# Two fused MLPs behind a dynamic convolution: steps 0 and 1 of the first MLP woven, closing products split around lone up parts

## The chip, the cores and the metric

The kernel runs on one core of a Trainium2 chip. The metric is the device time of one execution in microseconds, median of the runs.

## What is computed

A per-token convolution (softmax over 7 taps per head, 8 heads of 24 features), then two MLPs of 192 to 2048 to 192 features, the first with a leaky ReLU, the second with an ELU, over 8192 tokens:

```
w = softmax(weight_gen, axis=-1)                  # [2, 4096, 8, 7]
out[b,s,h,:] = sum_k w[b,s,h,k] * x_pad[b,s+k,h,:]  # x_pad: 6 zero rows ahead
x = out.reshape(8192, 192)
h = x @ moe_w_in;   g = maximum(0.01*h, h);            x = g @ moe_w_out
h = x @ moe2_w_in;  g = where(h > 0, h, exp(min(h, 0)) - 1);  out = g @ moe2_w_out
```

## The kernel before

Each f32 factor of a matrix product is held as two rounded parts, high and low (`*_hi`, `*_lo`), so that a product becomes three. The 192 features are held as 128 (`_a`) and 64 (`_b`); of the 64, the high part lies in partitions 0 to 63 and the low part in 64 to 127 of one tile `in_b`, and `in_b_up` holds the high part once more in the upper half. Most products use one half of TensorE's rows (LOW, HIGH), and two such, one in each half, run side by side: "a pair" here.

**Chunks, phases, steps.** Tokens come in 16 chunks of 512. A phase is one MLP on one chunk; the order is MLP 1 of chunk 0 (phase 0), MLP 1 of chunk 1 (phase 1), MLP 2 of chunk 0 (phase 2), and then in turn. A phase has 8 steps of 256 hidden features; step number g = 8 x phase + s. One step is an *up* part (up products into the PSUM bank pair `hidden[:, s % 2]`), an activation on ScalarE (line 1091 or 1093), a rounding to `hid_hi` on ScalarE (line 1109), the rest `hid_lo` on VectorE (line 1380), and three steps later a *down* part that adds into `y_a` and `y_b`.

**TensorE's order** is written out in `phase` (line 896). The up part has a first half (5 pairs) and a second half (4 pairs). The second half waits on `s_open` for the last product of the first, since both add to the same banks. In an ordinary step `down_open` (4 pairs) stands between the two halves, the second half is interleaved with down products, and `down_close` (line 766, 4 pairs) ends the step. In three steps the up part is *lone*, its halves back to back: steps 2, 8 and 10. Step 0 is `up_first` (line 669) and step 1 `up_whole` (line 695), in whole-array products. Ahead of step 8 stand the down part of step 5, the transposes of chunk 1's mix (line 877), and the whole down part of step 6 (`down_alone`, line 778).

**Waits that matter.** The up part of step g overwrites the bank pair of step g - 2: it waits for that step's activation (`s_leak`) where g - 2 is in `ASIDE` = (0, 1, 2, 9), and for its `hid_lo` (`s_lo` at least g - 1) otherwise. Step 0's `in_b` products wait at line 686 for `s_xin` 2 (VectorE, line 1299), step 8 at line 913 for `s_xin` 4 (VectorE, line 1302). In phase 0 a step with even s waits for the splits of its quarter of the up weights (`s_uplo`).

**Other engines.** ScalarE (line 1186 on): issues the load of `wk[1]`, two exponentials, packs, rounds the weight quarters 0 and 1 of `w_in` (`round_up`, lines 974 and 980), makes the input's high parts, rounds down weights (`round_down`, line 990), then runs the steps; `first_step` (line 1111) activates step 0 in two halves, rounds it and then rounds quarter 2. VectorE makes the mix of chunk 0 (`first_mixing`, line 1228; the newest tap is `product(6, prod, 0, J)`, line 1240), the low parts of inputs and weights, and every `hid_lo`. GpSimd makes the other mixes. SyncE's queue (line 443 on) loads `wk[0]`, the rows of `x`, waits for all of them (lines 449 and 450), loads quarters 0 and 1 of `w_in` and the first of `w_out`, and behind `s_termv` and `s_unpack` (lines 455 and 457) the rest.

Of the kernel before, what the change touches and what calls it, by code (L numbers as in the profile page):

```python
# [5 lines left out]
def attention_leaky_elu_mlps(  # L6
# [61 lines left out]
    with ctx:  # L68
# [345 lines left out]
        def _(sp):  # L414
# [28 lines left out]
            load_w(0)  # L443
            sp.dma_start(xw[:, PAD:, :], x_rows[:, 0:J * D].rearrange("p (j d) -> p j d", d=D)).then_inc(s_x0, 16)
# [155 lines left out]
        def _(pe):  # L600
# [68 lines left out]
            def up_first():  # L669

                def product(i, w, v, **flags):
                    return nc.tensor.matmul(hidden[:, 0, HALF[i]], w[0][:, i * P:(i + 1) * P], v[input_of(0, 0)][:, :], **flags)


                pe.wait_ge(s_xhi, 1)
                pe.wait_ge(s_uplo, 1)
                for i in (0, 1):
                    product(i, up_a_hi, in_a_hi, start=True, stop=False)
                    product(i, up_a_lo, in_a_hi, start=False, stop=False)

                pe.wait_ge(s_xin, 1)
                product(0, up_a_hi, in_a_lo, start=False, stop=False)
                product(1, up_a_hi, in_a_lo, start=False, stop=False)
# [3 lines left out]
                product(0, up_b_hi, in_b, start=False, stop=False)  # L687
                product(1, up_b_hi, in_b, start=False, stop=False)
                pe.wait_ge(s_uplo, 2)
                pe.wait_ge(s_xup, 1)  # L690
                low, high = up_pair(0, input_of(0, 0), 0, stop=True)
                low.then_inc(s_up1, 1)
                high.then_inc(s_up, 1)

            def up_whole(m, src, s):

                def product(i, w, v, **flags):
                    cols = slice((2 * s + i) * P, (2 * s + i + 1) * P)
                    return nc.tensor.matmul(hidden[:, s % 2, HALF[i]], w[m][:, cols], v[src][:, :], **flags)  # L699

                up_pair(m, src, s, start=True)
                for i in (0, 1):
                    product(i, up_a_hi, in_a_hi, start=False, stop=False)
                    product(i, up_a_lo, in_a_hi, start=False, stop=False)
                    product(i, up_a_hi, in_a_lo, start=False, stop=False)
                    product(i, up_b_hi, in_b, start=False, stop=True).then_inc(s_up if i else s_open, 1)
# [59 lines left out]
            def down_close(m, s, d):  # L766

                down_a(m, s, d, LOW, 0, 2)
                pe.wait_ge(s_ybfirst, d + 1)
                down_b(m, s, d, HIGH, 0, 0)  # L770
                down_a(m, s, d, LOW, 1, 0)
                down_b(m, s, d, HIGH, 0, 1)
# [716 lines left out]
```

## Time and profile before

| | |
|---|---|
| median of 3 runs | 1130.13 us (1129.84 to 1130.41) |
| the profiled execution | 1129.72 us |
| its span, first to last instruction | 1127.9 us |
| TensorE busy | 1119.7 us, 99% of the span |
| ScalarE, VectorE, GpSimd busy | 744.0, 624.5, 390.4 us |
| mean granted TensorE clock | 0.999 |

In the profile PE is TensorE (PEld its weight loads), ACT ScalarE, DVE VectorE, POOL GpSimd, SP SyncE. L609 is line 609 of the kernel. A matmul record lasts longer (0.39 us) than the distance to the next one, since they are pipelined: waits of TensorE are read from the distance between starts. What stands behind "<-" in brackets is the inferred releaser of an idle time, and can be another that ended at the same moment.

### The profile page before, as it was taken

The numbers are of one execution on the slowest core, as the hardware profiler recorded it, in microseconds if no ns is written. First come the engines' busy times: TensorE is split into PE (matmuls) and PEld (weight loads), VectorE is DVE, ScalarE is ACT, GpSimd is POOL, SyncE is SP. The second block draws the span as 40 slices with busy tenths as digits, with TensorE's granted clock in tenths as the row PEclk, the third lists the DMA queues.
The fourth block names the chain that finished last, engine by engine and source line by source line (L and its number), as shares of the span: only waits on it lengthen the run. The fifth ranks groups of instructions, "written<-read, shape, count | busy, mean of one in ns | idle before, by whom it ended". The sixth has DMA issues, their size and how long they took to land.

```text
span 1127.9 us, 22691 instructions
## 1 busy us (share of the span) xinstructions
PE 1119.7 (99%) x9794; PEld 921.8 (82%) x9794; DVE 624.5 (55%) x654; ACT 744.0 (66%) x837; POOL 390.4 (35%) x407
## 2 busy tenths in 40 slices
PE   8999999999999999999999999999999999999998
PEld 6888888888888888888888888888888888888886
DVE  8677547365463645636456364554736546363555
ACT  6577657576575766757567575765757657576676
POOL 6663622607135080440805317062260713500000
PEclk9999999999999999999999999999999999999999
DMA  5412020211202102021020201102021120110001
GB/s 173 119 50 85 17 81 15 82 29 29 82 1 82 29 28 83 1 82 29 29 82 3 88 22 57 54 19 83 11 82 29 29 82 2 43 29 29 15 1 57
DMA packets 46080, 54.88 MB, mean 49 GB/s; under 512 B 4254, under 2 KB 34718, under 8 KB 45980
## 3 DMA queue, kind: packets, MB, share of 16 engines
q1 hardware_dynamic: 45836, 53.30, 15.6%
q8 instruction: 78, 1.28, 0.5%
q14 instruction: 22, 0.18, 0.1%
q10 hardware_dynamic: 144, 0.11, 0.0%
HBM read 35.71 MB, written 17.69 MB: 47 GB/s over the span
## 4 chain that ended last, share of the span: by engine, by line
PE 98%; DVE 1%; ACT 0%; DMA 0%; issue 0%; DVEq 0%
PE y_a L730 31%; PE hidden L609 31%; PE y_b L713 21%; PE hidden L614 10%; PE hidden L665 5%; DMA wk<-in_weight_gen_dram 0%; PE hidden L699 0%; DVE prod L1233 0%; DVE act L1233 0%; PE y_b L856 0%; DVE mix L1233 0%; PE hidden L666 0%; DVE staged L1233 0%; DVE act L1236 0%; DVE raw_d L1233 0%
## 5 line engine op out<-in xcount | busy, mean ns | idle before, releaser
L730 PE MATMUL y_a<-hid_hi,dn 64*128 64x512 f32 x2048 | 625.5, 386 | 0.0
L730 PEld LDWEIGHTS y_a<-hid_hi,dn 64*128 64x128 f32 x2048 | 375.7, 184 | 40.0
L713 PE MATMUL y_b<-hid_hi,dn 64*128 64x512 f32 x1024 | 395.5, 386 | 0.0
L713 PE MATMUL y_b<-hid_lo,dn 64*128 64x512 f32 x1024 | 395.4, 386 | 0.0
L730 PE MATMUL y_a<-hid_lo,dn 64*128 64x512 f32 x1024 | 394.4, 386 | 0.0
L609 PE MATMUL hidden<-in_a_hi,up_a_hi 64*128 64x512 f32 x1016 | 294.1, 387 | 0.2
L609 PE MATMUL hidden<-in_a_lo,up_a_hi 64*128 64x512 f32 x1016 | 293.6, 386 | 0.0
L609 PE MATMUL hidden<-in_a_hi,up_a_lo 64*128 64x512 f32 x1016 | 293.6, 386 | 0.0
L614 PE MATMUL hidden<-in_b,up_b_hi 64*128 64x512 f32 x1016 | 293.6, 386 | 0.0
L1380 DVE TENSOR_TENSOR hid_lo<-hidden,hid_hi 128x1024 fp32r<-128x1024 f32 x124 | 151.6, 1222 | 255.0 <-ACT hid_hi L1109 255.0
L1380 DVE TENSOR_TENSOR hid_lo<-act,hid_hi 128x1024 fp32r<-128x1024 f32 x131 | 165.5, 1264 | 189.2 <-ACT hid_hi L1109 189.2
L1091 ACT ACTIVATE hidden<-hidden 128x1024 f32<-128x1024 f32 x124 | 125.0, 1008 | 196.0 <-PE hidden L614 196.0
L1093 ACT ACTIVATE act<-hidden 128x1024 f32<-128x1024 f32 x127 | 130.5, 1027 | 159.8 <-PE hidden L614 158.1
L384 POOL TENSOR_TENSOR mix<-xw,wk 128x384 f32<-128x384 f32 x30 | 26.5, 884 | 562.6 <-DVE wk L1287 562.5
L713 PEld LDWEIGHTS y_b<-hid_hi,dn 64*128 64x128 f32 x1024 | 188.4, 184 | 20.3 <-issue 0.2
L730 PEld LDWEIGHTS y_a<-hid_lo,dn 64*128 64x128 f32 x1024 | 188.5, 184 | 20.0
L713 PEld LDWEIGHTS y_b<-hid_lo,dn 64*128 64x128 f32 x1024 | 188.5, 184 | 19.9
L397 POOL TENSOR_TENSOR mix<-mix,prod 128x384 f32<-128x384 f32 x180 | 194.3, 1079 | 2.4
L1355 DVE SCALAR_TENSOR_TENSOR act<-act,hidden 128x1024 f32<-128x1024 f32 x129 | 155.6, 1206 | 45.7 <-ACT act L1098 45.3
L384 POOL TENSOR_TENSOR prod<-xw,wk 128x384 f32<-128x384 f32 (+1 forms) x182 | 171.9, 952 | 9.4
L609 PEld LDWEIGHTS hidden<-in_a_hi,up_a_hi 64*128 64x128 f32 x1016 | 140.4, 184 | 22.0 <-PE hidden L666 1.5
L614 PEld LDWEIGHTS hidden<-in_b,up_b_hi 64*128 64x128 f32 x1016 | 140.4, 184 | 19.9
(143 smaller groups left out, 1312.3 us busy)
## 6 DMA issues: line engine op xcount, KB each, us to landing
xw<-in_x_dram SPq DMA_DIRECT2D x14, 960.0 KB, 5.2
raw_b<-squares_out SPq DMA_DIRECT2D x60, 96.0 KB, 2.2
out_dram<-staged SPq DMA_DIRECT2D x15, 384.0 KB, 2.6
squares_in<-prod SPq DMA_DIRECT2D x56, 96.0 KB, 2.0
squares_out<-ya SPq DMA_DIRECT2D x15, 256.0 KB, 2.0
raw_a<-squares_in SPq DMA_DIRECT2D x14, 256.0 KB, 2.9
raw_d<-in_moe_w_out_dram SPq DMA_DIRECT2D x8, 384.0 KB, 3.4
squares_out<-yb SPq DMA_DIRECT2D x15, 128.0 KB, 2.2
```

What stands on the lines that cost most here:

```text
L384: product = ops.tensor_tensor(dst, src, w, ALU.mult)
L397: ops.tensor_tensor(mix[:, j0:j1, :], mix[:, j0:j1, :], terms[k % n][:, j0:j1, :], ALU.add).then_inc(done, 1)
L609: return nc.tensor.matmul(hidden[:, s % 2, HALF[i]], w[m][rows, cols], v[src][rows, :], start=start, stop=stop)
L614: return nc.tensor.matmul(hidden[:, s % 2, HALF[i]], up_b_hi[m][rows, cols], in_b[src][rows, :], start=False, stop=stop)
L665: low = nc.tensor.matmul(hidden[:, s % 2, HALF[0]], up_b_lo[m][LOW, cols], in_b[src][LOW, :], start=start, stop=stop)
L713: return nc.tensor.matmul(y_b[d // ST % 2][:, :], dn[m][rows, f, P:2 * P], v[rows, s % HB, HALF[i]], start=start, stop=stop)
L730: return nc.tensor.matmul(y_a[bank][:, :], dn[m][rows, f, w:w + P], v[rows, s % HB, HALF[i]], start=start, stop=stop)
L1091: nc.scalar.activation((act if g in ASIDE else hidden)[:, s % 2, :], hidden[:, s % 2, :], ACT.Prelu, alpha=SLOPE).then_inc(s_leak, 1)
L1093: nc.scalar.activation(act[:, s % 2, :], hidden[:, s % 2, :], ACT.Relu, scale=-1.0).then_inc(s_relu, 1)
L1355: nc.vector.scalar_tensor_tensor(out=a, in0=a, scalar=-1.0, in1=h, op0=ALU.add, op1=ALU.max).then_inc(done, 1)
L1380: nc.vector.tensor_tensor(hid_lo[:, s % HB, :], (act if m or g in ASIDE else hidden)[:, s % 2, :], hid_hi[:, s % HB, :].bitcast(f32), ALU. ...
```

## The change

- SyncE's queue issues the load of `wk[1]` directly behind that of `wk[0]`; ScalarE's queue no longer does.
- `up_first` and `up_whole` become `up_first_two`: the high-input products of step 1 stand ahead of the wait for `in_b`, the others behind step 0's last. Step 1's `b_lo` pair (`up_pair`) goes between the halves of step 2's up part and signals `s_up` for step 1.
- `down_close` can be issued in halves. Step 6's stands between the halves of step 8's up part; of step 7's the first half (2 pairs) stays in step 9 and the second (2 pairs) stands between the halves of step 10's.
- ScalarE rounds quarter 2 of the up weights ahead of step 0's activation instead of behind its rounding.

```diff
--- before.py
+++ after.py
@@ -441,6 +441,7 @@
 
 
             load_w(0)
+            load_w(1)
             sp.dma_start(xw[:, PAD:, :], x_rows[:, 0:J * D].rearrange("p (j d) -> p j d", d=D)).then_inc(s_x0, 16)
             sp.wait_ge(s_pad, 1)
             for to in HALO_ROWS:
@@ -666,44 +667,41 @@
                 high = nc.tensor.matmul(hidden[:, s % 2, HALF[1]], up_b_lo[m][HIGH, cols], in_b_up[src][HIGH, :], start=start, stop=stop)
                 return low, high
 
-            def up_first():
-
-                def product(i, w, v, **flags):
-                    return nc.tensor.matmul(hidden[:, 0, HALF[i]], w[0][:, i * P:(i + 1) * P], v[input_of(0, 0)][:, :], **flags)
-
+            def up_first_two():
+                src = input_of(0, 0)
+
+                def product(s, i, w, v, **flags):
+                    cols = slice((2 * s + i) * P, (2 * s + i + 1) * P)
+                    return nc.tensor.matmul(hidden[:, s, HALF[i]], w[0][:, cols], v[src][:, :], **flags)
+
+                def a_hi(s):
+                    for i in (0, 1):
+                        product(s, i, up_a_hi, in_a_hi, start=True, stop=False)
+                        product(s, i, up_a_lo, in_a_hi, start=False, stop=False)
+
+                def a_lo(s):
+                    for i in (0, 1):
+                        product(s, i, up_a_hi, in_a_lo, start=False, stop=False)
 
                 pe.wait_ge(s_xhi, 1)
                 pe.wait_ge(s_uplo, 1)
-                for i in (0, 1):
-                    product(i, up_a_hi, in_a_hi, start=True, stop=False)
-                    product(i, up_a_lo, in_a_hi, start=False, stop=False)
-
+                a_hi(0)
                 pe.wait_ge(s_xin, 1)
-                product(0, up_a_hi, in_a_lo, start=False, stop=False)
-                product(1, up_a_hi, in_a_lo, start=False, stop=False)
+                a_lo(0)
+                a_hi(1)
 
                 pe.wait_ge(s_uphi, 2)
                 pe.wait_ge(s_xin, 2)
-                product(0, up_b_hi, in_b, start=False, stop=False)
-                product(1, up_b_hi, in_b, start=False, stop=False)
+                for i in (0, 1):
+                    product(0, i, up_b_hi, in_b, start=False, stop=False)
                 pe.wait_ge(s_uplo, 2)
                 pe.wait_ge(s_xup, 1)
-                low, high = up_pair(0, input_of(0, 0), 0, stop=True)
+                low, high = up_pair(0, src, 0, stop=True)
                 low.then_inc(s_up1, 1)
                 high.then_inc(s_up, 1)
-
-            def up_whole(m, src, s):
-
-                def product(i, w, v, **flags):
-                    cols = slice((2 * s + i) * P, (2 * s + i + 1) * P)
-                    return nc.tensor.matmul(hidden[:, s % 2, HALF[i]], w[m][:, cols], v[src][:, :], **flags)
-
-                up_pair(m, src, s, start=True)
-                for i in (0, 1):
-                    product(i, up_a_hi, in_a_hi, start=False, stop=False)
-                    product(i, up_a_lo, in_a_hi, start=False, stop=False)
-                    product(i, up_a_hi, in_a_lo, start=False, stop=False)
-                    product(i, up_b_hi, in_b, start=False, stop=True).then_inc(s_up if i else s_open, 1)
+                a_lo(1)
+                product(1, 0, up_b_hi, in_b, start=False, stop=False)
+                product(1, 1, up_b_hi, in_b, start=False, stop=False).then_inc(s_open, 1)
 
             def down_b(m, s, d, rows, i, n):
 
@@ -763,13 +761,16 @@
                 down_a(m, s, d, LOW, 0, 1)
                 down_a(m, s, d, HIGH, 1, 2)
 
-            def down_close(m, s, d):
-
-                down_a(m, s, d, LOW, 0, 2)
-                pe.wait_ge(s_ybfirst, d + 1)
-                down_b(m, s, d, HIGH, 0, 0)
-                down_a(m, s, d, LOW, 1, 0)
-                down_b(m, s, d, HIGH, 0, 1)
+            def down_close(m, s, d, halves=(0, 1)):
+
+                if 0 in halves:
+                    down_a(m, s, d, LOW, 0, 2)
+                    pe.wait_ge(s_ybfirst, d + 1)
+                    down_b(m, s, d, HIGH, 0, 0)
+                    down_a(m, s, d, LOW, 1, 0)
+                    down_b(m, s, d, HIGH, 0, 1)
+                if 1 not in halves:
+                    return
                 down_a(m, s, d, LOW, 1, 1)
                 down_b(m, s, d, HIGH, 1, 0)
                 down_a(m, s, d, LOW, 1, 2)
@@ -896,8 +897,9 @@
             def phase(m, c, ph, dm, dc):
                 for s in range(ST):
                     g = ST * ph + s
-                    if known(ph) and g == 0:
-                        up_first()
+                    if g == 0:
+                        up_first_two()
+                    if g < 2:
                         continue
                     of, step = (dm, ST - LAG + s) if s < LAG else (m, s - LAG)
                     if ph == 1 and s == 0:
@@ -907,7 +909,9 @@
                         transpose_mix(1, 1)
 
                         pe.wait_ge(*down_split(0, DN_PARTS - 1))
-                        down_alone(0, ST - 2, g - 2)
+                        pe.wait_ge(s_lo, g - 1)
+                        down_open(0, ST - 2, g - 2)
+                        down_middle_apart(0, ST - 2, g - 2)
                     if s == 0:
 
                         pe.wait_ge(s_min if m else s_xin, 2 * (c + 1))
@@ -931,10 +935,14 @@
                     elif of_two == 1:
 
                         pe.wait_ge(s_g, ST * c_two + (s - 2) % ST + 1)
-                    if ph == 0 and s == 1:
-                        up_whole(m, input_of(m, c), s)
-                        continue
                     up(m, input_of(m, c), g, s, False)
+                    if g == 2:
+
+                        up_pair(0, input_of(0, 0), 1, stop=True)[1].then_inc(s_up, 1)
+                    if (ph, s) == (1, 0):
+                        down_close(0, ST - 2, g - 2)
+                    if (ph, s) == (1, 2):
+                        down_close(0, ST - 1, g - 3, (1,))
                     if (ph, s) in ((0, 2), (1, 0), (1, 2)):
                         up(m, input_of(m, c), g, s, True)
                         continue
@@ -955,7 +963,7 @@
                     else:
                         up(m, input_of(m, c), g, s, True)
                         down_middle_apart(of, step, d)
-                    down_close(of, step, d)
+                    down_close(of, step, d, (0,) if (ph, s) == (1, 1) else (0, 1))
 
             sum_first_mix()
             run(pe, phase)
@@ -1114,7 +1122,6 @@
                     nc.scalar.activation(act[:, 0, HALF[i]], hidden[:, 0, HALF[i]], ACT.Prelu, alpha=SLOPE).then_inc(signal(s_leak, s_leak1, i), 1)
                 act_e.wait_ge(s_leak1, 1)
                 rounding(0, 0, 0, 0)
-                round_up(0, 2)
 
             def last_step():
                 s = ST - 1
@@ -1183,7 +1190,6 @@
                         if (ph, s) in DN2_AT:
                             round_down(1, DN2_AT.index((ph, s)))
 
-            act_e.dma_start(wk[1][:, :, :], w_rows[:, J * H * TAPS:2 * J * H * TAPS].rearrange("p (a k) -> p a k", k=TAPS)).then_inc(s_w[1], 16)
             softmax_exp(0)
             softmax_exp(1)
 
@@ -1196,6 +1202,7 @@
             mlp1_input_hi(0, 1)
             round_up_b(0, 1)
             round_down(0, 0)
+            round_up(0, 2)
             run(act_e, phase)
             take_y(1, CH - 1, LAST)
             stage_last()
```

## Rows read from the trace of the kernel before

**Rows 1.** Stretches: us, busy PE, PEld, DVE, ACT, POOL, clock, DMA, GB/s.

```profile
61.70:1115.00 1053.30, 1053.30 (x9296) 870.70 (x9294) 570.67 (x587) 699.27 (x773) 353.67 (x364) 1.00 0.14 43
```

**Rows 2.** Timeline, TensorE, steps 0 to 3: start, us, line, output<-inputs, count.

```profile
16.84 0.73 PE L672 MATMUL hidden<-in_a_lo,up_a_hi 128*128 128x512 f32 x2
17.82 0.71 PE L672 MATMUL hidden<-in_b,up_b_hi 128*128 128x512 f32 x2 [0.25 <-ACT up_b_hi L980]
...
21.19 0.51 PE L609 MATMUL hidden<-in_a_hi,up_a_hi 64*128 64x512 f32 x2
...
22.70 0.50 PE L609 MATMUL hidden<-in_a_hi,up_a_hi 64*128 64x512 f32 x2
23.04 0.39 PE L609 MATMUL hidden<-in_a_hi,up_a_lo 64*128 64x512 f32 x2
...
23.74 0.39 PE L609 MATMUL hidden<-in_a_hi,up_a_hi 64*128 64x512 f32 x2
```

**Rows 3.** Timeline, VectorE, 4 to 40 us.

```profile
4.49 0.42 DVE L1264 TENSOR_REDUCE wsum<-soft 128x32 f32<-128x256 f32 x1 [0.16 <-ACT soft L1000]
...
14.13 0.68 DVE L1213 TENSOR_TENSOR up_a_lo<-raw_a,up_a_hi 128x512 fp32r<-128x512 f32 x1
...
16.82 0.86 DVE L1299 TENSOR_TENSOR in_b<-y_a,in_b 64x256 fp32r<-64x256 f32 x2
...
22.48 1.88 DVE L1380 TENSOR_TENSOR hid_lo<-act,hid_hi 128x1024 fp32r<-128x1024 f32 x1
...
30.36 1.22 DVE L1380 TENSOR_TENSOR hid_lo<-hidden,hid_hi 128x1024 fp32r<-128x1024 f32 x1 [0.47 <-ACT hid_hi L1109]
...
33.26 1.35 DVE L1213 TENSOR_TENSOR up_a_lo<-raw_a,up_a_hi 128x512 fp32r<-128x512 f32 x1
...
35.54 1.21 DVE L1380 TENSOR_TENSOR hid_lo<-hidden,hid_hi 128x1024 fp32r<-128x1024 f32 x1
```

**Rows 4.** Timeline, TensorE, into step 6.

```profile
36.48 0.39 PE L730 MATMUL y_a<-hid_lo,dn 64*128 64x512 f32 x1
...
36.90 0.50 PE L609 MATMUL hidden<-in_a_hi,up_a_hi 64*128 64x512 f32 x2
```

**Rows 5.** Timeline, TensorE, step 8, its two halves.

```profile
52.33 0.39 PE L665 MATMUL hidden<-in_b,up_b_lo 64*128 64x512 f32 x1
...
52.78 0.50 PE L609 MATMUL hidden<-in_a_hi,up_a_hi 64*128 64x512 f32 x2
```

**Rows 6.** Timeline, ScalarE, 14 to 34 us.

```profile
17.61 0.83 ACT L990 ACTIVATE dn<-raw_d 128x768 fp32r<-128x768 f32 x1
18.99 1.09 ACT L1114 ACTIVATE act<-hidden 128x512 f32<-128x512 f32 x2 [0.56 <-PE hidden L665]
...
21.14 0.61 ACT L974 ACTIVATE up_a_hi<-raw_third 128x512 fp32r<-128x512 f32 x1
...
24.46 1.03 ACT L1091 ACTIVATE act<-hidden 128x1024 f32<-128x1024 f32 x1 [0.18 <-DVE hid_lo L1380]
```

**Rows 7.** Timeline, SyncE's queue, 5 to 17 us.

```profile
6.86 0.34 SPq L421 DMA_DIRECT2D raw_a<-in_moe_w_in_dram  x1
...
13.70 1.26 SPq L427 DMA_DIRECT2D ya<-in_moe_w_in_dram  x2
```

**Rows 8.** The chain that ended last, its beginning: start, us, what.

```profile
0.72 2.48 DMA wk<-in_weight_gen_dram
...
5.82 1.99 DVE prod L1233 x3
```

**Rows 9.** Issue to landing: into ya at 12 to 17, wk after 60.

```profile
DMA to landing us min/median/max: 4.6/4.7/4.7
...
DMA to landing us min/median/max: 2.1/2.6/3.1
```

**Rows 10.** Timeline, VectorE, 46 to 60 us.

```profile
50.05 0.68 DVE L1302 TENSOR_TENSOR in_b<-hidden,in_b 64x512 fp32r<-64x512 f32 x1
56.12 1.22 DVE L1380 TENSOR_TENSOR hid_lo<-hidden,hid_hi 128x1024 fp32r<-128x1024 f32 x1 [5.39 <-ACT hid_hi L1109]
```

## The prediction

> **What bounds the kernel now.** I read the stretches first. From 61.7 to 1115 us TensorE is busy in every microsecond, at a granted clock of 1.00 [rows 1]. The change edits nothing in that stretch and nothing in the tail, and the stretch has no idle time to give. Both differences can only come from the first 61.7 us, and reach the end only as a shift of the whole stretch. So I asked, gap by gap, what ends each TensorE gap before 61.7 us, and whether that thing moves.
>
> Then the timeline of TensorE alone. In a run without a wait a pair of half-array products starts every 0.2275 us and a whole-array one every 0.235 us. After a wait the first one holds the second back to 0.34 us (22.70 to 23.04), 0.11 us more than the step: I call this the refill. Five gaps matter:
> - 17.82: the second of the two low-half products that start at 16.84 is due at 17.08, so the next was due at 17.31. Wait 0.51, refill about 0.09 [rows 2]. The profile hints at ScalarE's `up_b_hi`, but line 686 waits for `s_xin` 2, which VectorE's `in_b` subtraction gives at 16.82 + 0.86 = 17.68 [rows 3].
> - 22.70: step 2's second half waits for its own first half (`s_open`). The first half starts at 21.19, its fifth pair at 22.24; 22.70 is 0.46 later, so 0.23 of wait and 0.11 of refill [rows 2].
> - 36.90: step 6. The pair before started at 36.48, 0.42 earlier, so 0.19 of wait, and a refill of about 0.07 [rows 4]. This one is of another kind: step 6 needs `s_lo` 5, the rest of step 4, which VectorE starts at 35.54 and ends at 36.75 [rows 3].
> - 52.78: step 8's second half after its fifth pair at 52.33: 0.45, so 0.22 + 0.11 = 0.33 [rows 5].
> - the same again in step 10, two steps on, at the same size (0.33).
>
> **What sets 36.90** decides the first half of the change. Backwards on VectorE: 35.54 stands directly behind weight splits (33.26 and others) that follow 30.36, and 30.36 waits for ScalarE's `hid_hi` of step 3. ScalarE comes to that without a pause from 24.46 (activation of step 2, three roundings of weights, step 3), and 24.46 waits for VectorE's first `hid_lo` at 22.48 + 1.88 = 24.36, which stands in an unbroken VectorE queue back to the first product of the mix [rows 3, 6]. No link of this chain is a TensorE product of steps 0 to 2. So what TensorE gains before 24 us it waits for at 36.90.
>
> **The change part by part.**
>
> *wk[1]'s load moves from ScalarE's queue to SyncE's, second in order.* The x load and the halo loads are issued one issue later, about 0.4 us (SyncE's issues in [rows 7] take 0.34 and 0.63). SyncE issues the first MLP weights at 6.86, once the halo has landed; the VectorE product that needs it is the third of the group that starts at 5.82 and ends at 7.81, a quarter of a product long and so at about 7.4 [rows 7, 8]. With 0.4 the halo is there by 7.26: hidden, just. wk[1] would land about 1.13 + 2.6 = 3.7, and at the longest landing seen (3.1) at 4.2; VectorE takes it up just before 4.0 and has 0.16 us idle before 4.49 [rows 3], so it costs 0 to 0.16. wk[0] shares the engines with it less. Its landing took 2.48 and starts the critical chain; later loads of the same size took 2.1 to 3.1 [rows 8, 9]. So this part is worth between -0.38 and +0.16 on everything. I take -0.05, near nothing, because most of the 2.48 is common to all landings. The DMA page of the Trainium skill (DMA: Bandwidth & Descriptors, "Issuing engines are not separate DMA queues") says that transfers from either queue run on the same 16 engines interleaved, and that a second issuer saves only sequencer time. By that the part would be worth nothing but the 0.4 us of issue; no row here shows the two orders side by side.
>
> *Step 1 woven into step 0.* Four high-half products of step 1 (4 x 0.235 = 0.94) go into the 0.51 us wait before 17.82. The two `in_b` products of step 0 then start at 17.31 + 0.94 = 18.25, 0.43 later, and lose their refill, so step 0's result comes about 0.35 later and ScalarE's activation could start at 18.99 + 0.35 = 19.34 [rows 2, 6]. On TensorE alone the work behind is 0.60 us earlier. The switches between whole and half array are three before and three after, so they cancel.
>
> *round_up(0, 2) ahead of step 0 on ScalarE.* After `dn` at 17.61 (0.73 to the next) the two roundings start at 18.34 and 18.87, if the loads are there. The last of the third quarter's loads is issued at about 14.33 (the second of 13.70's pair) and lands 4.6 later, 18.95 [rows 7, 9]. So the second starts at 18.95 and ScalarE is free at 18.95 + 0.53 = 19.48 (call it S), or 19.9 if the landing slips with the 0.4 us of SyncE. The two halves of step 0's activation take 1.09, and TensorE sees them at S + 1.14.
>
> *Step 2 and the end of step 1.* Step 2's first half, due by TensorE at about 20.3, waits for that: S + 1.14 = 20.6 (before 21.19). Its fifth pair starts 1.05 later, step 1's last pair at +1.28 (it fills the `s_open` wait: gain 0.34), so `s_up` 2 gives ScalarE step 1 at S + 1.14 + 1.28 + 0.42 = S + 2.84. That takes 1.03, and step 3 needs it (`s_leak` 2): TensorE goes on at S + 3.89 = 23.4, before 23.74 [rows 2]. A gain of 0.34 is left of 0.94 (0.60 + 0.34), the rest turned into two new waits for ScalarE. ScalarE itself then rounds step 1 from S + 3.87 for 0.97, and is ready for step 2's activation at S + 4.84 = 24.32, against 24.46 where VectorE releases it [rows 6]. So the chain to 36.90 stays put with 0.14 us to spare; with S = 19.9 it slips by 0.28. I take +0.05, bounds 0 and +0.33. The 0.34 us that TensorE gained are waited for at 36.90.
>
> *Step 8: down_close of step 6 between the halves.* The four closing pairs fill 0.33 us. But they used to stand ahead of step 8's first half, and covered the wait for `s_xin` 4. That first half started at 52.33 - 4 x 0.2275 = 51.42; without four pairs ahead it is due at 50.51, while VectorE's `in_b` ends at 50.05 + 0.68 = 50.73 and reaches TensorE 0.05 to 0.14 later [rows 5, 10]. Both hang on the transposes of the second mix, so the distance is fixed whatever happens before. New wait about 0.30, new refill 0.11: 0.41 spent for 0.33 gained, net about +0.07. Bounds: -0.33 (no wait) and +0.2.
>
> *Step 10: half of down_close of step 7.* Two pairs fill the gap, 0.46 for 0.45, so the 0.33 is gained. The first half comes two pairs earlier, from about 58.15 (52.78 + 23 pairs and a refill) to 57.7; it needs the rest of step 8, 56.12 + 1.22 = 57.34 [rows 10], 0.3 us to spare. Net -0.33, at the worst -0.2. `s_dn` 7 and 8 come up to 2 us later; their readers (ScalarE's copy of `y_a` after step 9 and TensorE's step 11) come later still.
>
> Sum: -0.05 + 0.05 + 0.07 - 0.33 = **-0.26 us**. The profiled execution took 1129.72 (span 1127.9 and 1.8 around it); it would take 1129.46. The median of the runs lies 0.41 above that execution: **1129.9 us**. All lower ends together give -1.04, all upper ends +0.49.
>
> **The rivals.**
> - *The weave pays in full.* Every filled gap stays filled: -(0.60 + 0.34 + 0.33 + 0.33) = -1.6, 1128.5 us. For it: TensorE is the busy engine. Against it: 35.54 and 50.05, two VectorE rows that no edit moves [rows 3, 10]. Chance 0.07.
> - *No new wait in step 8*, otherwise as forecast: -0.26 - 0.40 = -0.66, 1129.5. It needs 50.73 to be early by 0.3. Chance 0.10.
> - *VectorE and GpSimd fall otherwise into step.* The same subtraction of 128x512 took 0.68 before GpSimd's mix ran, and 1.35 beside it at 33.26 [rows 3]; the chain to 36.75 has several such. A shift of hundredths at the start may change who waits, one such step being worth 0.67 either way: 1129.2 or 1130.5. The Trainium skill (SBUF — State Buffer, "SBUF: two separate sides") says that the pair of ports which the two share is an exclusive lock, held for a whole instruction by whoever starts first; by that the trace's 1.35 for 0.68 is one such wait. Chance 0.13.
> - *Slower: ScalarE stands behind a late third quarter.* The rounding is now queued ahead of step 0's activation, which TensorE's steps 2 and 3 and VectorE's `hid_lo` wait for. Beyond 0.14 us of delay of the landing at 18.95, each microsecond goes to 36.90 in full, and to the end. With the other terms at -0.31 it decides the sign from 0.45 us of delay. Loads of one kind differ by 1.0 between shortest and longest (2.1 to 3.1, [rows 9]); 1.0 later gives -0.31 + 0.86 = +0.55, 1130.7. Passing 0.2% would need 2.7 us. For it: SyncE's issues before it start 0.4 later and all share the engines. Against it: line 455 holds the third quarter until VectorE has read the first rows, so it is itself issued when it was. Chance 0.15.
> - *The words say more than the diff.* That VectorE makes the whole newest tap is in the kernel before already (line 1240 covers all rows), so nothing moves by it. It costs nothing and takes no chance of its own.
>
> **Chances and range.** Forecast 0.55 (1129.4 to 1130.4). The executions before spread from 1129.84 to 1130.41, 0.3 about their median; bounds and spread give 1128.9 to 1131.0. About 0.2%, 2.26 us, is what a measurement can tell from no change. Nothing here reaches it: there is 0.94 + 0.26 + 0.66 us of gap to win, and 2.7 us of delay needed to lose. Faster 0.02, same 0.95, slower 0.03.
>
> **What would show it.** Right: step 6 starts within 0.3 of 36.90 behind a longer TensorE wait; step 8's first half starts near 50.8 behind a wait of 0.3; step 11 starts about 0.26 earlier than now, and so does everything to the end. ScalarE rounds the third quarter at 18.3 to 19.5. Wrong: step 6 starts at 36.5 or earlier (the VectorE chain didn't hold), no wait at 50.8, or ScalarE waits for a load between 18.4 and 20.

## The result, and the profile after

| | before | changed |
|---|---|---|
| median | 1129.95 us (22 runs) | 1131.40 us (22 runs) |
| lowest, highest | 1129.68, 1131.56 | 1130.19, 1134.49 |
| profiled execution | 1129.72 | 1130.31 |
| its span | 1127.9 | 1128.5 |

The ratio is 1.0014, with a 95% interval of 1.0008 to 1.0019: slower by 1.5 us, inside the 0.2% that were called "same", but outside the range of 1128.9 to 1131.0. And the changed kernel spreads: its shortest run is 0.5 us above that of before, its longest 2.9 us. Two questions follow: where the profiled execution lost 0.6 us, and what the others lost on top.

ScalarE in the changed kernel, from step 0 to step 2 (what answers to [rows 6]):

```profile
17.25 0.83 ACT L998 ACTIVATE dn<-raw_d 128x768 fp32r<-128x768 f32 x1
18.47 0.63 ACT L982 ACTIVATE up_a_hi<-raw_third 128x512 fp32r<-128x512 f32 x1 [0.39 <-DMA raw_third<-in_moe_w_in_dram]
19.59 0.63 ACT L988 ACTIVATE up_b_hi<-ya 128x512 fp32r<-128x512 f32 x1 [0.49 <-DMA ya<-in_moe_w_in_dram]
20.25 1.09 ACT L1122 ACTIVATE act<-hidden 128x512 f32<-128x512 f32 x2
...
23.14 1.03 ACT L1099 ACTIVATE act<-hidden 128x1024 f32<-128x1024 f32 x1 [0.65 <-PE hidden L667]
...
25.16 1.01 ACT L1099 ACTIVATE act<-hidden 128x1024 f32<-128x1024 f32 x1
```

TensorE at step 2's first and second half, step 3, into step 6, step 8's first half and step 12 (answering to [rows 2, 4, 5]):

```profile
21.43 0.51 PE L610 MATMUL hidden<-in_a_hi,up_a_hi 64*128 64x512 f32 x2 [1.29 <-ACT act L1122]
...
22.93 0.50 PE L610 MATMUL hidden<-in_a_hi,up_a_hi 64*128 64x512 f32 x2
...
24.22 0.50 PE L610 MATMUL hidden<-in_a_hi,up_a_hi 64*128 64x512 f32 x2
...
37.08 0.39 PE L728 MATMUL y_a<-hid_lo,dn 64*128 64x512 f32 x1
...
37.43 0.50 PE L610 MATMUL hidden<-in_a_hi,up_a_hi 64*128 64x512 f32 x2
...
51.32 0.50 PE L610 MATMUL hidden<-in_a_hi,up_a_hi 64*128 64x512 f32 x2
...
65.26 0.50 PE L610 MATMUL hidden<-in_a_hi,up_a_hi 64*128 64x512 f32 x2
```

and VectorE (answering to [rows 3, 10]; the first line is the one that waits for the very first load):

```profile
2.86 0.39 DVE L1280 TENSOR_REDUCE wmax<-wk 128x32 f32<-128x224 f32 x1 [1.48 <-DMA wk<-in_weight_gen_dram]
...
31.04 1.23 DVE L1387 TENSOR_TENSOR hid_lo<-hidden,hid_hi 128x1024 fp32r<-128x1024 f32 x1 [1.52 <-ACT hid_hi L1117]
...
36.08 1.21 DVE L1387 TENSOR_TENSOR hid_lo<-hidden,hid_hi 128x1024 fp32r<-128x1024 f32 x1
...
50.58 0.69 DVE L1309 TENSOR_TENSOR in_b<-hidden,in_b 64x512 fp32r<-64x512 f32 x1
...
63.98 1.23 DVE L1387 TENSOR_TENSOR hid_lo<-hidden,hid_hi 128x1024 fp32r<-128x1024 f32 x1 [1.46 <-ACT hid_hi L1117]
```

Read in order of time, against the kernel before:

- The first load is taken up at 2.86 instead of 3.22: 0.36 us gained, and TensorE's step 0 starts 0.36 earlier too (15.42 for 15.78).
- ScalarE stands twice for the third quarter (0.39 and 0.49 us idle) and starts step 0's activation at 20.25. The quarter comes in several loads. The first part (`raw_third`, 256 KB) is taken up at 18.47, the last (into `ya`) at 19.59, and it is the last that decides when ScalarE is free. TensorE has nothing to do meanwhile: 1.29 us idle ahead of step 2. This wait for a load between 18.4 and 20 is one of the three signs of being wrong that the prediction names.
- ScalarE then stands 0.65 us more for step 1's last pair (L667), which the change put behind step 2's first half.
- Step 2's activation starts at 25.16, where it was 24.46. It carries through ScalarE's unbroken queue to the `hid_hi` that VectorE waits for (31.04 for 30.36), to VectorE's 36.08 (35.54) and so to step 6: 37.43 for 36.90, +0.53.
- From step 6 to step 11 the closing products gain 0.29 (60.79 for 60.55).
- Step 12 starts at 65.26, for 64.88: behind a wait that the kernel before doesn't have. The lag of 0.22 us that was left just ahead of it grows to 0.38 at its start and, with the slower restart behind the wait, to 0.55 at step 13; so nearly all of the 0.29 is lost again. From step 13 on the distance is 0.55 to 0.59 up to the end.

### The profile page after: what moved, and what is told of

It is laid out like the page before. It is cut to its first block, busy times and chain, and to the rows that moved or that the text cites. A ratio compares the mean times of both kernels' runs of the same rounds, so it can differ in the third digit from the quotient of the medians.

```text
span 1128.5 us, 22691 instructions
## 1 busy us (share of the span) xinstructions
PE 1118.9 (99%) x9794; PEld 922.3 (82%) x9794; DVE 623.9 (55%) x654; ACT 744.3 (66%) x837; POOL 389.9 (35%) x407
## 4 chain that ended last, share of the span: by engine, by line
PE 97%; DVE 1%; DMA 1%; ACT 0%; SPq 0%; issue 0%; DVEq 0%
PE y_a L728 31%; PE hidden L610 31%; PE y_b L711 20%; PE hidden L615 10%; PE hidden L666 5%; DMA ya<-in_moe_w_in_dram 0%; DMA wk<-in_weight_gen_dram 0%; DVE prod L1240 0%; DVE act L1240 0%; PE hidden L667 0%; ACT act L1122 0%; ACT act L1099 0%; DVE mix L1240 0%; DVE staged L1240 0%; DVE raw_d L1240 0%
```

## The experiments

Each kernel was timed beside runs of the kernel before on the same chip; their medians were 1129.94 (e1 to e4), 1129.93 (a2 to e7), 1129.82 (e8 to e11) and 1129.88 (e12, a3). The intervals of single ratios are about 0.1% to either side, so 1 us between medians is near the limit: only the ratios of the changed kernel and of e5, e6 and e12 lie clear of 1. The steps inside a trace are read to hundredths, but each is one execution. "Low clock" below counts runs whose mean granted clock is 0.998 or less. That mark alone doesn't prove a fall in mid-kernel: in the kernel before the clock stands at 0.50 from about 1126 us on, behind the last product, so a late last store lowers the mean too, and the four marked runs of that kernel are all long ones (1131.22 to 1131.68). A mean of 0.997 or less stands in 6 of the 44 runs of the changed kernel and in none of the 115.

The columns on the third quarter give moments in the profiled execution: when the load of its first part is issued and has landed, and when its last part has landed. The next one tells when ScalarE starts step 0's activation.

| kernel | median, lowest to highest | low clock | first part issued, landed | last part landed | step 0's activation | step 6 starts |
|---|---|---|---|---|---|---|
| before (115 runs beside the experiments) | four medians 1129.82 to 1129.94, runs 1129.66 to 1131.72 | 4 of 115 | 12.70, 17.77 | 19.02 | 18.99 | 36.90 |
| changed (result) | 1131.40, 1130.19 to 1134.49 | 9 of 22 | 12.38, 18.45 | 19.57 | 20.25 | 37.43 |
| changed (a2) | 1131.42, 1130.22 to 1132.22 | 2 of 11 | 12.52, 19.47 | 20.24 | 20.92 | 38.34 |
| changed (a3) | 1131.79, 1130.04 to 1132.99 | 5 of 11 | 14.30, 18.43 | 19.20 | 19.87 | 37.19 |
| e1 | 1129.73, 1129.43 to 1130.79 | 0 of 11 | 12.71, 18.42 | 19.57 | 19.43 | 37.03 |
| e2 | 1129.64, 1129.36 to 1130.65 | 0 of 11 | 12.50, 18.79 | 19.84 | 18.72 | 36.61 |
| e3 | 1129.84, 1129.69 to 1131.58 | 2 of 11 | 14.47, 18.48 | 19.15 | 19.83 | 36.93 |
| e4 | 1130.58, 1130.27 to 1131.30 | 0 of 11 | 14.83, 18.72 | 19.38 | 20.06 | 37.76 |
| e5 | 1133.69, 1132.55 to 1134.98 | 6 of 6 | 12.62, 18.72 | 20.19 | 21.91 | 40.08 |
| e6 | 1131.31, 1130.37 to 1132.07 | 0 of 11 | 12.35, 18.44 | 19.61 | 20.29 | 37.46 |
| e7 | 1129.31, 1129.06 to 1131.02 | 0 of 11 | 12.27, 19.45 | 20.15 | 19.00 | 36.60 |
| e8 | 1130.54, 1129.78 to 1132.71 | 0 of 11 | 12.74, 19.20 | 20.16 | 20.83 | 38.76 |
| e9 | 1130.45, 1129.93 to 1131.55 | 0 of 11 | 12.46, 19.16 | 19.94 | 20.62 | 37.55 |
| e10 | 1129.54, 1129.36 to 1131.55 | 0 of 11 | 12.50, 18.54 | 19.66 | 19.22 | 36.82 |
| e11 | 1129.99, 1129.83 to 1131.61 | 1 of 11 | 14.20, 18.39 | 18.93 | 19.44 | 37.05 |
| e12 | 1132.28, 1131.85 to 1133.24 | 0 of 11 | 14.22, 18.58 | 19.67 | 21.78 | 39.18 |

In e3, e11, e12 and a3 the first part is issued at 14.2 to 14.5 instead of 12.3 to 12.7. SyncE waits there for `s_unpack`, which the last but one group of TensorE's transposes of chunk 0's mix gives, and in these four TensorE works at half pace at first. The first eight transposes of `prod`, in the kernel before and in a3:

```profile
6.93 1.13 PE L856 MATMUL y_b<-ident,prod 128*128 128x128 f32 x8 [0.86 <-DVE prod L1233]
```

```profile
7.08 2.05 PE L857 MATMUL y_b<-ident,prod 128*128 128x128 f32 x8 [1.01 <-DVE prod L1240]
```

The traces' record of the granted clock begins, at 1.00, only at 10.3 to 10.9 us in these four, and at 4.3 to 7.4 in the other twelve. (The stretches of the profile show 1.00 where there is no record.) A later issue doesn't mean a later landing: in e3, e11 and a3 the last part landed earlier than in most others (18.93 to 19.20), in e12 at 19.67.

**Which part costs: e1 to e4.** e1 puts the rounding back behind step 0:

```diff
-            round_up(0, 2)
             run(act_e, phase)
 ...
                 rounding(0, 0, 0, 0)
+                round_up(0, 2)
```

> The changed kernel, but ScalarE rounds the third quarter of the up weights behind step 0 again. Theory Q (ScalarE stands behind a late load): the chain on VectorE that sets step 6 holds again and keeps the 0.36 us that the first load gained, so step 6 starts near 36.55, the end comes about 0.3 us earlier than in the kernel before, and the runs lie within 0.5 us of each other at a clock of 0.999. Theory W (the woven products and their own new waits cost it): the time stays 0.6 to 1.5 us above the kernel before. Theory L (one queue for all loads delays them): also stays above.

Measured: 1129.73 and a spread of 1.4 us, for the 0.5 expected. Moving that one call back takes the 1.5 us away, weave and all. So the loss doesn't come about without the rounding ahead; W and L fall as causes by themselves, but not yet as parts of it (see e9). Step 6 is at 37.03, not at the expected 36.55, although the first load was taken up 0.53 us early (2.69). In this execution `wk[1]`, now behind it, landed late, and VectorE stood 0.56 us for it:

```profile
2.69 0.39 DVE L1280 TENSOR_REDUCE wmax<-wk 128x32 f32<-128x224 f32 x1 [1.31 <-DMA wk<-in_weight_gen_dram]
...
4.07 0.39 DVE L1454 TENSOR_REDUCE top<-wk 128x32 f32<-128x224 f32 x1 [0.56 <-DMA wk<-in_weight_gen_dram]
```

e2 is the kernel before with the load alone:

```diff
             load_w(0)
+            load_w(1)
```

> The kernel before with wk[1] loaded by SyncE behind wk[0], nothing else. Theory Q: 0.36 us faster than before (the first landing 2.1 instead of 2.5 us), narrow runs. Theory L: no faster or slower, with a spread of some us as in the changed kernel.

Measured: 1129.64, 0.3 below before, and 0.26 in the trace up to TensorE's last products. As theory Q expected, though the interval of the ratio (0.9988 to 1.0005) includes no gain and the runs spread over 1.3 us.

e3 is the kernel before with the rounding ahead alone (e1's diff the other way round):

> The kernel before with the third quarter's rounding ahead of step 0 on ScalarE, nothing else. Theory Q: step 0's activation starts when the load has landed and is rounded, at 19.5 us or later instead of 18.99; with the landing of the kernel before (18.95) step 6 moves by under 0.2 us, each later landing by its lateness, so the median is 0 to 0.8 above before and the runs spread over a microsecond or more. Theory W: no change at all, since nothing is woven.

Measured: 1129.84, the same as before. In its profiled execution the first part landed at 18.48, no earlier than in the changed kernel (18.45), but ScalarE came to it only at 18.58, since the first load of all had gained nothing; the last part was there at 19.15. Step 0's activation started at 19.83 and step 6 at 36.93. So the call alone costs nothing here, although step 0 comes 0.84 us later. That execution took 1131.11 all the same, and shows one way in which a run gets near 1131.2: up to 1112 us it lies 0.05 behind before, and its last store took 3.3 us to land where before it was 2.0. (The 2.3 in the first line below is the store at 1116 us.) In the profiled executions of e8 and e5 the last store took 3.1 and 3.6, in the other thirteen 2.0 to 2.1. The times from issue to landing of the stores from 1115 us on, in the kernel before:

```profile
DMA to landing us min/median/max: 1.9/2.0/2.3
```

and in e3:

```profile
DMA to landing us min/median/max: 2.2/2.3/3.3
```

e4 holds the third quarter's loads until later, in the changed kernel:

```diff
             sp.wait_ge(s_unpack, 1)
+            sp.wait_ge(s_uplo, 1)
```

> The changed kernel with the third quarter's loads held until VectorE has split the first one, issued near 14.5 instead of 12.4 us. Theory Q: they land about 2 us later, ScalarE stands for them, step 6 starts near 39.5, and the time is 1132.4 or more; if the long runs of the changed kernel also come from this wait, then their lower clock (0.996 to 0.998) shows in more of these runs. Theory W: no change against the changed kernel (1131.4).

Measured: 1130.58, and this expectation was wrong. Issued over 2 us later, the first part landed after 3.9 us instead of 6.1, and was taken up at 18.75, hardly later than in the changed kernel (18.47); the last part landed 0.2 earlier (19.38). That the loads spend the difference in a queue behind those issued before them fits this, but isn't shown. The wait ahead of step 2 was 0.79, and no run had a low clock. Step 6 came at 37.76 all the same, later than in the changed kernel's 37.43: VectorE's first `dn` subtraction after step 3 (L410), which ran beside GpSimd's mix, took 0.94 us for 0.42.

**The two parts together: e8 and e9.** e8 is the changed kernel with `wk[1]` on ScalarE's queue again, e9 the kernel before with the load and the rounding ahead, nothing woven and no closing products moved.

> The changed kernel with wk[1] issued on ScalarE's queue again. Theory Q+L (the rounding ahead of step 0 costs because the loads behind wk[1] on SyncE land later): the third quarter's first part lands near 17 to 18 us as in the kernel before instead of 18.4 to 19.5, ScalarE hardly stands for it, the first landing is back at 2.5 us, and the time is 1129.9 to 1130.3 with no clock under 0.999. Theory Q alone (the third quarter is late whatever the order): 1131.4 and a spread as in the changed kernel.

Measured: 1130.54, between the two theories. Its profiled execution had the last part land at 20.16 though `wk[1]` wasn't ahead on SyncE. So a late quarter doesn't need that order: with `wk[1]` on ScalarE the last part landed at 18.93, 19.02, 19.15 and 20.16 in four kernels, on SyncE at 19.20 to 20.24 in eleven executions (e4, which issues it later, aside). The order may make it later on average; that stays open. The profiled execution took 1132.71, the longest of its runs: step 0's activation at 20.83, the subtraction L410 beside GpSimd 1.03 us long, so step 6 at 38.76, and a last store of 3.1 us. 5 of 11 runs were at 1130.2 or less, against 2 of 44 below 1130.2 of the changed kernel.

> The kernel before with two parts of the change: wk[1] on SyncE and the third quarter's rounding ahead of step 0; nothing woven, no closing products moved. Theory Q+L: the two together bring most of the loss, 1130.4 to 1131.4, by a later step 6, though each alone cost nothing. TensorE's wait ahead of step 2 is shorter by the products of step 1 that it still has (about 0.9 us), so fewer runs have a clock under 0.999 than of the changed kernel. Theory W: within 0.2 us of before.

Measured: 1130.45. The pair goes with 0.6 us more at the median, though e2 alone gained and e3 alone cost nothing. The interval of the ratio (0.9993 to 1.0010) doesn't carry that, but 10 of the 11 runs lie above 1130.2, for 7 of the 33 beside them, and the trace ends 0.64 later. TensorE's wait ahead of step 2 was 0.81, and no run had a low clock.

So the pair brings less than half of the 1.5 us, and not most of it. The trace shows what the weave adds. Here, without it, ScalarE goes from step 0's rounding to step 1's activation without a pause, and VectorE takes up step 3's rest at 30.65:

```profile
22.77 1.00 ACT L1092 ACTIVATE act<-hidden 128x1024 f32<-128x1024 f32 x1
...
30.65 1.23 DVE L1380 TENSOR_TENSOR hid_lo<-hidden,hid_hi 128x1024 fp32r<-128x1024 f32 x1 [1.01 <-ACT hid_hi L1110]
```

From step 0's activation to step 2's it takes 4.15 us (20.62 to 24.77). In the three profiled executions of the changed kernel it takes 4.90 to 4.92, because ScalarE stands 0.63 to 0.65 us for step 1's last pair. So the weave, harmless by itself (e11 below), costs by this comparison 0.75 us once step 0's activation is late enough to set the pace. VectorE is here only 0.29 us later than before (30.65 for 30.36), with step 0's activation at 20.62; in the changed kernel it was 0.68 later with 20.25. The other 0.36 of e9's 0.65 at step 6 came on VectorE, where L410 took 0.93 us beside GpSimd for 0.42.

**The clock: e5, e6 and e12, beside the changed kernel itself (a2, a3).**

> The changed kernel itself, once more, beside the three below. About half of its 22 runs so far lie at 1130.2 to 1130.5, the others up to 1134.5 at a clock of 0.996 to 0.998. The same is expected here, median 1130.4 to 1131.8.

Measured: 1131.42. Its profiled execution (1131.42) is a typical one, and shows the same mechanism at a later landing (first part 19.47, last 20.24). ScalarE:

```profile
19.49 0.63 ACT L982 ACTIVATE up_a_hi<-raw_third 128x512 fp32r<-128x512 f32 x1 [1.45 <-DMA raw_third<-in_moe_w_in_dram]
20.26 0.63 ACT L988 ACTIVATE up_b_hi<-ya 128x512 fp32r<-128x512 f32 x1
20.92 1.08 ACT L1122 ACTIVATE act<-hidden 128x512 f32<-128x512 f32 x2
```

and TensorE ahead of step 2:

```profile
22.10 0.51 PE L610 MATMUL hidden<-in_a_hi,up_a_hi 64*128 64x512 f32 x2 [2.00 <-ACT act L1122]
```

1.45 us of ScalarE standing, 2.00 us of TensorE idle, step 6 at 38.34, TensorE's last products 1.46 later than before, with the clock at 1.00 up to there. So this alone can bring a run to the median. Since a late last store does so too, which share of the runs near 1131.3 belongs to which stays open.

e5 makes the wait longer with work for ScalarE that nobody needs:

```diff
+            for n in range(3):
+                nc.scalar.activation(up_a_hi[0][:, cols2], raw_up(0, 2)[0][:, :], ACT.Copy).then_inc(s_extra, 1)
+                act_e.wait_ge(s_extra, n + 1)
             round_up(0, 2)
```

> The changed kernel with ScalarE's rounding of the third quarter's first part done three more times (about 0.65 us each) ahead of step 0's activation, so that TensorE's wait ahead of step 2 grows by about 1.3 us. Theory Q with idle TensorE as the cause of the long runs: step 6 comes 1.3 us later, the shortest runs are at 1131.6, and more of the runs than of the changed kernel show a clock under 0.999 and 1 to 4 us on top. Rival D (the long runs are late loads alone, the clock has nothing to do with it): the extra work on ScalarE covers late loads, so the runs come closer together, near 1131.6.

Measured: 1133.69, every run at a low clock. The trace shows it: stretches of one microsecond (columns as in [rows 1]), and TensorE's pairs in them:

```profile
22.00:23.00 1.00, 0.00 (x0) 0.00 (x0) 0.20 (x1) 0.99 (x2) 1.00 (x2) 1.00 0.21 68
23.00:24.00 1.00, 0.91 (x8) 0.90 (x10) 0.00 (x0) 0.92 (x1) 0.92 (x2) 1.00 0.53 63
24.00:25.00 1.00, 1.00 (x10) 0.72 (x8) 0.82 (x1) 0.26 (x2) 1.00 (x2) 0.75 1.05 347
25.00:26.00 1.00, 1.00 (x6) 0.74 (x6) 1.00 (x2) 0.97 (x2) 1.00 (x2) 0.50 0.00 0
```

```profile
23.09 0.50 PE L611 MATMUL hidden<-in_a_hi,up_a_hi 64*128 64x512 f32 x2 [2.93 <-ACT act L1123]
...
25.17 0.63 PE L611 MATMUL hidden<-in_a_hi,up_a_lo 64*128 64x512 f32 x2
25.59 0.63 PE L611 MATMUL hidden<-in_a_lo,up_a_hi 64*128 64x512 f32 x2
26.02 0.63 PE L616 MATMUL hidden<-in_b,up_b_hi 64*128 64x512 f32 x2
```

After 2.93 us of waiting, TensorE works at the full clock for 1.4 us, and then at 0.50, the lower of its two levels, 1.2 GHz: pairs start every 0.42 to 0.43 us instead of 0.23. Seven pairs in a row (25.17 to 27.73) start so before the clock comes back at about 27.9.

e6 leaves the changed kernel's waits alone and gives TensorE five products to do in the one ahead of step 2; their result is read by nobody:

```diff
+                for _ in range(5):
+                    nc.tensor.matmul(y_b[1][:, :], up_a_hi[0][:, 0:P], in_a_hi[src][:, :], start=True, stop=True)
```

> The changed kernel with five whole-array products on TensorE (1.2 us) that nobody reads, in the wait ahead of step 2. Theory idle TensorE: nothing is delayed, the clock stays at 0.999 or above in all runs, and the runs over 1131.5 vanish; median near 1130.4. Rival D: the same spread as the changed kernel, since the loads land as before.

Measured: 1131.31, and no run with a low clock; TensorE's wait shrank to 0.27. Half the expectation held. The clock loss went, but the median stayed, since the late quarter is still there (last part 19.61, step 6 at 37.46 in its profile). On this chip only 2 of 11 runs of the changed kernel itself had a low clock, so e6 alone proves little. Hence e12, e5's roundings and eleven such products:

> The kernel of e5 (three more roundings ahead of step 0 on ScalarE) with eleven whole-array products on TensorE that nobody reads, 2.6 us, in the wait ahead of step 2. ScalarE's delay is that of e5, TensorE's idle time nearly none. Theory (the idle stretch costs clock): no run under 0.999, shortest runs near those of e5 less the 0.7 to 1.3 us of clock, median 1131.5 to 1132.2. Rival (the delay alone makes e5's time): median 1133.7 as in e5.

Measured: 1132.28 for 1133.69, and 0 of 11 runs with a low clock for 6 of 6. ScalarE's delay is the same in both (step 0's activation at 21.78 and 21.91); TensorE works instead of waiting, and the clock stays:

```profile
24.00:26.00 2.00, 1.91 (x16) 1.13 (x14) 1.95 (x2) 1.34 (x3) 1.92 (x3) 1.00 0.54 177
```

So it is the idle stretch that costs the clock, not the delay. The loss is 1.4 us at the median here; between the two traces it is 0.8 at TensorE's last products (3.05 and 2.24 behind before), and e5's profiled execution also had a late last store. The median of 1132.28 lies just above the expected 1131.5 to 1132.2.

> The changed kernel once more beside e12, for the clock of its runs: of 33 so far 12 have a mean clock of 0.998 or less, and those are 1131.65 us and more. Expected: 2 to 6 of 11; if the profiled one is among them, its clock falls to 0.50 between the wait ahead of step 2 and step 4.

Measured: 1131.79, 5 of 11 with a low clock. The profiled execution was the shortest of all, 1130.04: the last part landed at 19.20, ScalarE started step 0's activation at 19.87 without standing for the first part, TensorE waited 0.36, step 6 began at 37.19. Even this one is 0.29 behind the kernel before at step 6. No profile caught a run of the changed kernel with a low clock. That its clock falls in this same place is therefore concluded, from e5, e6 and e12 and from its idle times of 1.3 and 2.0 us, and not seen. Against it speaks e8: its profile has a wait of 1.47 us in that place, and none of its 11 runs a low clock.

**The weave and the closing products: e11, e10, e7.** e11 is the kernel before with the weave alone.

> The kernel before with the weave alone: step 1's products into step 0 and its last pair between the halves of step 2; wk[1] on ScalarE, third quarter behind step 0, no closing products moved. Theory (VectorE's chain sets step 6): step 2 and 3 start earlier, step 6 stays at 36.9 behind a longer wait, and the time is that of before within 0.1 us. Rival (the weave pays or costs): more than 0.3 us either way.

Measured: 1129.99 beside 1129.82. Step 2's second half starts at 22.09 instead of 22.70, step 3 waits 0.41 us for ScalarE, and VectorE's rest of step 4, at 35.70, sets step 6 at 37.05:

```profile
23.68 0.50 PE L609 MATMUL hidden<-in_a_hi,up_a_hi 64*128 64x512 f32 x2 [0.41 <-ACT act L1092]
...
37.05 0.50 PE L609 MATMUL hidden<-in_a_hi,up_a_hi 64*128 64x512 f32 x2
```

Nothing gained at step 6, as forecast; the median lies 0.17 above before and the trace ends 0.16 later, for the 0.1 expected. e10 is the changed kernel with the rounding behind step 0 and step 6's down part whole again ahead of step 8; e7 is e10 with one more edit, which rounds the second MLP's second weight quarter behind step 10 instead of step 9:

```diff
-        UP2_AT = [(1, 0), (1, 1), (1, 5), (1, 7)]
+        UP2_AT = [(1, 0), (1, 2), (1, 5), (1, 7)]
```

> The kernel of e7 without the move of the second MLP's second weight quarter: third quarter behind step 0, step 6's closing products as before, step 7's closing half still between the halves of step 10. Theory: step 12 waits for the rest of step 10 behind ScalarE's queue, a TensorE wait near 64.5 us that e7 doesn't have, so 0.1 to 0.3 us slower than e7 (1129.31), about 1129.5. Rival (step 12 not bound there): equal to e7.

> The changed kernel with the third quarter's rounding behind step 0, the down part of step 6 whole ahead of step 8 as before, and the second MLP's second weight quarter rounded one step later (behind step 10 rather than step 9). Theory Q: VectorE's chain sets step 6 as in the kernel before, less what the first load gained (0.2 to 0.4), step 12 no longer waits behind that quarter on ScalarE, so step 10's 0.33 us stay: 0.5 to 0.7 us faster than before, 1129.3. Rival: step 12 isn't bound by ScalarE's queue, then 0.2 to 0.3 faster only, with a TensorE wait left at 65 us.

Measured: 1129.54 and **1129.31**. Step 12 in e10:

```profile
64.58 0.50 PE L610 MATMUL hidden<-in_a_hi,up_a_hi 64*128 64x512 f32 x2
```

and in e7:

```profile
64.24 0.39 PE L610 MATMUL hidden<-in_a_hi,up_a_hi 64*128 64x512 f32 x2
```

The 0.50 is the mark of a first product after a wait, 0.39 that of one in a run. Without the quarter ahead of it on ScalarE the rest of step 10 is there early, and step 10's 0.33 us stay to the end: e7 lies 0.64 us ahead of before in the trace and 0.6 at the median. Its ratio to before, 0.9993, has an interval of 0.9984 to 1.0002, so the trace carries that claim more than the timing does. It is the fastest kernel of the study by its median.

## Why the prediction was wrong

- **The landing of the third quarter** is the step that failed, with its term of +0.05 (0 to +0.33). "lands 4.6 later, 18.95" was one execution's number (and the lowest of three; that load took 4.67 and landed at 19.02), taken as the value, with the slip bounded at 0.4 us. In the changed kernel the last part landed at 19.20, 19.57 and 20.24, in all sixteen executions at 18.93 to 20.24, and the term measured +0.29, +0.53 and +1.44 at step 6. The mechanism was right. The rival "ScalarE stands behind a late third quarter" had it, with the price of one microsecond for each; with a chance of 0.15 it was the main case. The spread of 1.0 us that it took came from other loads, in a stretch where the DMA engines were busy 0.14 of the time [rows 1, 9]; the 1.3 us seen here isn't far from that. The mistake was to take the landing of the kernel before as the middle.
- **The slack of 0.14 us** wasn't there. ScalarE starts step 0's activation 0.66 us after it takes up the last rounding (19.59 to 20.25), and not 0.53, and "S + 4.84" measured 4.91, 4.92 and 4.90. With these, a landing at 19.02 gives 24.6 for step 2's activation, 0.1 behind the 24.46 of before. "S + 4.84" holds the weave's 0.75 us; the prediction didn't set it against the path without the weave, where e9 needed 4.15. The weave was weighed for what it gives TensorE, and its price on ScalarE's path went unseen.
- **The slack at step 12** was never looked at. I followed step 10's 0.33 as far as step 11. The rest of step 10 ends at 64.59 in the kernel before, step 12 starts at 64.88, so 0.24 us were to be had, in a queue of ScalarE that starts with step 9 and doesn't move; a wait takes 0.05 of the 0.29. It is the same question as for step 6, and I asked it only there. e10 against e7 shows the wait.
- **The clock** was given no case. All rows were at 1.00 and I had the new waits at under 0.5 us; they became 0.4, 1.3 and 2.0 in the three profiles. Up to a third of the runs (16 of 44) pay for it, 6 by the stricter mark of 0.997.
- **VectorE and GpSimd falling otherwise into step** was a rival at 0.13, and it showed: in e4, e8 and e9 the subtraction L410 took 0.93 to 1.03 us for 0.42. In the first two profiles of the changed kernel it took 0.42 and 0.50, so it isn't the loss there.
- Right, point by point: VectorE's chain holds step 6, the weave gains nothing there (e11); the new wait in step 8 (51.32 where 51.04 was due, 0.28 for "about 0.30"), and steps 8 and 10 together give 0.29 for 0.26; the halo is hidden.
- Mis-sized, both ways: the first load was worth 0.34 to 0.53, at and past the bound of 0.38, and not 0.05. And `wk[1]`, bounded at 0.16, cost VectorE 0.56 us of idle time in e1; it landed at 3.2 to 4.2. VectorE takes it up between 0.45 earlier (a2) and 0.26 later (a3) than before, so the part could also lose. The first two loads are of one size and were issued within 0.01 us of each other. Issued one after the other, the first lands 0.3 to 0.5 us earlier. The rule of the Trainium skill that was weighed in the prediction (DMA: Bandwidth & Descriptors, "Issuing engines are not separate DMA queues"), that the transfers of two issuers interleave on the same engines, agrees with that. What was wrong is my reading of it, that nothing would be gained.

## What to carry to other kernels

Work put ahead of the critical step on an in-order engine is free only while its inputs are there; before moving it, take the moment at which its last load has landed from several executions, not from one, above all for loads issued among many others. Compare moments, and not times from issue to landing: in these traces a load issued 2 us later took 2 us less. And look at what else the change puts on the path behind that step: the weave cost nothing alone and 0.75 us here. After following a gain to the next wait, follow it past that one as well, to the first step whose releaser doesn't move with it. An idle stretch of TensorE can cost more than its length, since the clock may fall after it: shown here for 2.9 us, inferred for 1.3 to 2.0. A few products that nobody reads kept it up.

## What the runs showed of the hardware

- One load of 256 KB: issued at 12.3 to 12.7 us it took 5.1 to 7.2 us to its landing (eleven executions), issued at 14.2 to 14.8 it took 3.9 to 4.4 (five). It landed between 17.8 and 19.5 either way.
- TensorE did its first transposes at half pace in four of sixteen executions (eight of them in 2.05 us instead of 1.13), and the record of the full clock began at 10.3 to 10.9 us in these four, at 4.3 to 7.4 in the others. It moved the issue of a load by nearly 2 us.
- TensorE's clock fell to 0.50 about 1.4 us after work had been taken up again (at 23.09), not during the wait of 2.93 us (e5), and came back at about 27.9 us. Idle times of 0.8 us (e4, e9) and of 1.47 (e8) went with no low clock in 33 runs.
- The last store takes 2.0 to 2.1 us to land in thirteen executions and 3.1 to 3.6 in three (e8, e3, e5). It is one reason why a part of the runs of the kernel before lie near 1131.2.
